# A float32 attention and two MLPs on one core: the early tensors and the second MLP's weights move from the bottom to the top of SBUF

## The reference, cut to what matters

```
q, k, v: (2, 6080, 256) float32; tau: scalar
w_in: (256, 2048), w_out: (2048, 256), once for each of two MLPs

qn = q / (norm(q, axis=1) + 1e-6);  kn = k / (norm(k, axis=1) + 1e-6)
a  = softmax(kn.transpose(0, 2, 1) @ qn / tau)     # 256 x 256 for each batch
x  = (v @ a).reshape(12160, 256)
x  = relu(x @ w_in1)**2 @ w_out1
return relu(x @ w_in2)**2 @ w_out2
```

## Time and profile before

| | |
|---|---|
| median of 3 runs | 2197.22 us (2196.81 to 2197.89) |
| the profiled execution's own time | 2196.81 us |
| its span, first to last instruction | 2194.7 us |
| mean granted TensorE clock | 0.998 |
| TensorE busy | 2179.6 us, 99% |
| VectorE, ScalarE busy | 1252.9 us (57%), 1018.1 us (46%) |

### The profile page before, as it was taken

The page is one execution under the profiler, slowest core; times in us unless marked ns, Lnnn a source line. Parts: engine busy times, 40 slices in busy tenths (PEclk is TensorE's granted clock), DMA queues, the critical chain, the costliest instruction groups (busy, mean ns, idle before and its releaser), DMA issues.

```text
span 2194.7 us, 29614 instructions
## 1 busy us (share of the span) xinstructions
PE 2179.6 (99%) x9836; PEld 1826.6 (83%) x9836; DVE 1252.9 (57%) x1875; ACT 1018.1 (46%) x1722; POOL 3.2 (0%) x10
## 2 busy tenths in 40 slices
PE   8999999999999999999999999999999999999998
PEld 7888888888888888888888888888888888888887
DVE  6765555555565555656655555555555555555544
ACT  5554444444444454444544444444444444444443
POOL 0000000000000000000000000000000000000000
PEclk9999999999999999999999999999999999999999
DMA  8310001100011000112111010110110101101001
GB/s 294 96 49 20 19 19 25 33 19 19 19 29 29 19 19 20 33 23 49 37 20 19 1 20 0 19 19 0 19 18 1 19 0 19 19 0 18 10 1 19
DMA packets 215874, 60.94 MB, mean 28 GB/s; under 512 B 199281, under 2 KB 203377, under 8 KB 215825
## 3 DMA queue, kind: packets, MB, share of 16 engines
q1 hardware_dynamic: 215824, 60.31, 11.7%
HBM read 47.84 MB, written 12.45 MB: 27 GB/s over the span
## 4 chain that ended last, share of the span: by engine, by line
PE 99%; DVE 0%; DMA 0%; ACT 0%; issue 0%; DVEq 0%; SPq 0%
PE bank L321 32%; PE bank L323 32%; PE bank L322 32%; PE bank L455 2%; PE bank L402 0%; DMA qk<-in_k 0%; PE bank L416 0%; DVE s_acc L818 0%; PE bank L410 0%; DVE stats L822 0%; DVE rawl L713 0%; DVE out_sb L726 0%; ACT s_acc L592 0%; ACT rawh L521 0%; DVEq L90 0%
## 5 line engine op out<-in xcount | busy, mean ns | idle before, releaser
L747 DVE TENSOR_TENSOR g_sb<-r_sb 128x512 f32<-128x512 f32 (+1 forms) x768 | 527.3, 687 | 896.6 <-ACT r_sb L545 890.4
L545 ACT ACTIVATE r_sb<-bank 128x512 f32<-128x512 f32 (+1 forms) x768 | 456.0, 594 | 1109.3 <-PE bank L323 1102.1
L713 DVE TENSOR_TENSOR gl<-g_sb,gh 128x512 fp32r<-128x512 f32 (+1 forms) x768 | 519.7, 680 | 0.5 <-DVE g_sb L747 0.5
L533 ACT ACTIVATE gh<-r_sb 128x512 fp32r<-128x512 f32 (+1 forms) x768 | 470.7, 619 | 0.0
L321 PE MATMUL bank<-yh,w2h 128*128 128x512 f32 (+1 forms) x768 | 297.8, 388 | 0.0
L321 PE MATMUL bank<-xh,w1h 128*128 128x512 f32 (+1 forms) x768 | 297.4, 387 | 0.0
L322 PE MATMUL bank<-yl,w2h 128*128 128x512 f32 (+1 forms) x768 | 297.4, 387 | 0.0
L322 PE MATMUL bank<-xl,w1h 128*128 128x512 f32 (+1 forms) x768 | 297.4, 387 | 0.0
L321 PE MATMUL bank<-gh,o2h 128*128 128x512 f32 (+1 forms) x768 | 297.3, 387 | 0.0
L323 PE MATMUL bank<-yh,w2l 128*128 128x512 f32 (+1 forms) x768 | 297.3, 387 | 0.0
L323 PE MATMUL bank<-gh,o2l 128*128 128x512 f32 (+1 forms) x768 | 297.3, 387 | 0.0
(11 more groups left out here) (101 smaller groups left out, 1623.8 us busy)
## 6 DMA issues: line engine op xcount, KB each, us to landing
v_sb<-in_v SPq DMA_DIRECT2D x88, 128.0 KB, 3.0
out<-out_sb SPq DMA_DIRECT2D x88, 128.0 KB, 2.5
raw<-in_q SPq DMA_DIRECT2D x22, 256.0 KB, 2.7
raw<-in_k SPq DMA_DIRECT2D x22, 256.0 KB, 3.0
qk<-in_q SPq DMA_DIRECT2D x10, 512.0 KB, 5.2
qk<-in_k SPq DMA_DIRECT2D x10, 512.0 KB, 6.3
w_early<-in_moe_w_in SPq DMA_DIRECT2D x4, 512.0 KB, 6.0
xT<-in_moe_w_out SPq DMA_DIRECT2D x4, 512.0 KB, 3.9
```

The source lines that it names most:

```text
L533: nc.scalar.activation(gh[:, f % SLOTS, 0:n], r_sb[:, f % 2, 0:n], ACT.Square).then_inc(gh_done, 1)
L545: nc.scalar.activation(r_sb[:, f % 2, 0:n], h_ps[f % SLOTS][:, 0:n], ACT.Relu)\
L713: return nc.vector.tensor_tensor(dst, x, as32(hi), ALU.subtract)
L747: nc.vector.tensor_tensor(g_sb[:, f % 2, 0:n], r, r, ALU.mult).then_inc(sq_done, 1)
```

## The change

One block of allocations is moved behind another. The instructions are the same, row for row, on each engine: 3354 on TensorE, 704 on VectorE, 654 on ScalarE, 14 on GpSimd and 118 on SyncE as the program holds them (loops once), and so are their waits. Only the byte addresses in them differ.

```diff
-        QS, SQ = 4, 2
-        with ExitStack() as early:
-            qk = [sb(f"qk{n}", [P, 2, J * C], scope=early) for n in range(QS)]
-            qk_squares = [sb(f"qk_squares{n}", [P, 2, J * C], scope=early) for n in range(SQ)]
-            w_early = sb("w_early", [P, PIECES, PIECE], scope=early)
-        w2h, w2l = sb("w2h", [P, CB, F], f32r), sb("w2l", [P, CB, F], f32r)
-        o2h, o2l = sb("o2h", [P, NF, C], f32r), sb("o2l", [P, NF, C], f32r)
         w1h, w1l = sb("w1h", [P, CB, F], f32r), sb("w1l", [P, CB, F], f32r)
         o1h, o1l = sb("o1h", [P, NF, C], f32r), sb("o1l", [P, NF, C], f32r)
         xh, xl = sb("xh", [P, CB, TILE], f32r), sb("xl", [P, CB, TILE], f32r)
...
         tau_sb, rtau = stats[:, 0:1], stats[:, 1:2]
         neg_max, row_sum = stats[:, 2:4], stats[:, 4:6]
 
+        QS, SQ = 4, 2
+        with ExitStack() as early:
+            qk = [sb(f"qk{n}", [P, 2, J * C], scope=early) for n in range(QS)]
+            qk_squares = [sb(f"qk_squares{n}", [P, 2, J * C], scope=early) for n in range(SQ)]
+            w_early = sb("w_early", [P, PIECES, PIECE], scope=early)
+        w2h, w2l = sb("w2h", [P, CB, F], f32r), sb("w2l", [P, CB, F], f32r)
+        o2h, o2l = sb("o2h", [P, NF, C], f32r), sb("o2l", [P, NF, C], f32r)
         weights = {"A": (w1h, w1l, o1h, o1l), "B": (w2h, w2l, o2h, o2l)}
```

## The result

The changed kernel takes 2223.77 us, the median of 4 runs (2222.77 to 2223.85), against 2197.01 for the kernel before in 4 runs. The ratio is 1.0121, 95% interval 1.0107 to 1.0136: slower by 26.8 us, where no change was forecast.

What follows compares the result with a forecast made beforehand. TensorE, by the distances between matmul starts, was taken to bound the kernel. Three address terms summed 0 + 0 + 0 against the profiled 2196.81 us, giving a forecast median of 2197.2 us, range 2195.8 to 2198.8.

Steps and rivals of the forecast that it cites:

- The reading of the bound: Whole run: TensorE busy 2179.6 of 2194.7 us, so time is the sum of distances between matmul starts plus 15.1 us.
- The first term: Stages A and B: w1h to o1l and xh to stats move down 65,536 bytes with the same remainders; cost 0.
- The third: Start of the run: first loads of q and k to multiples of 256; taken as 0, bounds -0.3 to +0.6 us.
- The change, part by part: Step pricing three groups of moved addresses, with no instruction added, removed or moved; sum 0 + 0 + 0.
- A faster load gains nothing. Cost: 0: Stages B: w2h to o2l move to the top, on multiples of 256; weight loads are not on the path, 0.
- 106 ns said to be spare: MLP stages: a load takes at most 120 ns and has 226.6 ns to hide in.
- place does not matter: MLP matmuls: w1l and w2l groups share a 389 ns median, so time shows no dependence on where weights are.
- rival (a): Stages B faster: the weights' 128-byte offset may cost 13.3 ns per matmul; 56 us and about 5 more, 2136 us; chance 0.03.
- the forecast of 0.94: Whole kernel: chance given to no measurable change, within about 0.2%, 4.4 us.
- a load is hidden: MLP stages: weight loads hide behind running matmuls with 106 ns to spare, and hidden loads do not stretch a matmul.
- Rival (c): Stages B slower: weight loads of 240 ns would set the matmul distance; 57 us, 2254 us; chance 0.01.
- Rival (b): From 14 to 44 us: slower loads of q and k set the pace; at 25% longer 2203.6 us; chance 0.02.

Runs made afterwards that it cites:

- e9: Kernel before with pads so that only w2l and o2l, low weights of the second MLP, lie 128 bytes off the moving operands; 2215.22 us, ratio 1.0083.
- e2: Kernel before with 128 unused bytes ahead of everything, so every tensor starts on a multiple of 256; 2197.65 us, ratio 0.9998.
- e1: Changed kernel with 128 unused bytes ahead of the early tensors, so w2h to o2l stay at the top, 128 past a multiple of 256; 2196.75 us, ratio 0.9999.
- e11: Kernel before, but the middle matmul of each MLP three uses 64 weight columns, half of that product left out; 2222.75 us in one execution.
- e3: Kernel before with 128 unused bytes ahead of the early tensors and of w1h, so only w2h to o2l start on a multiple of 256; 2223.78 us, ratio 1.0123.
- e5: Kernel before with 128 unused bytes between the weights and xh, so the MLPs' moving operands start on a multiple of 256; 2247.06 us, ratio 1.0225.
- e10: Kernel before with 128 unused bytes ahead of and behind xl, yl and gl, so only these lie 128 off the weights; 2224.57 us, ratio 1.0119.
- e8: Kernel before with pads ahead of w1h and xh, weights 192 bytes past the moving operands in A, 224 in B, modulo 256; 2238.71 us, ratio 1.0194.
- e13: Kernel before with pads ahead of w1h and xh, weights 64 bytes past the moving operands in A, 192 in B, modulo 256; 2234.31 us, ratio 1.0167.

## Why the prediction was wrong

The reading of the bound held: the run is the sum of distances between matmul starts, and 5.7 ns on half of them are the result. The first term (w1h to o1l and the moving operands go down by 65,536 bytes, 0 us) held: A stages kept their pace but for 1.8 us at the borders to B. The third (first loads, -0.3 to +0.6 us) can't be read off the one profile of the changed kernel. The first matmul starts at 4.66 and the DMA share is 0.95 again, but the matmuls of q and k (L455) take 41.3 us and not 40.4, ScalarE's wait for the last tile is 2.36 us and not 2.05, the norms wait 0.24 us for VectorE, and the fold begins 0.8 us later, which is over the upper bound. Most of it lies between 8.6 and 10.7 us, where TensorE started 12 matmuls before and 6 now. That this is the lower clock is likely and not shown: the records of the granted clock begin at 8.5 us before and at 10.8 us now. It is not tied to the addresses: in `e9`, whose early tensors lie where they lay before, it is 6 matmuls too, the q and k matmuls take 41.2 us and the fold begins at 56.87; in `e2`, whose early tensors start on a multiple of 256, they take 40.2 us and it begins at 56.04. With the remainder restored at the same top place (`e1`) the median is 0.6 us under its own before. By all this the term is 0 within the spread of the runs, as forecast.

The rule of the Trainium skill, DMA: Bandwidth & Descriptors, section "How a descriptor splits into AXI transactions", that the prediction named showed no gain for the writes here: 2784 pieces of 4,096 bytes take 159 ns in the median, before and after.

The step that failed is the second, "The change, part by part": "A faster load gains nothing. Cost: 0", with 106 ns said to be spare. It measured +24.6 us (24.1 and 0.5), in the distances of the B matmuls. Two inferences in it were wrong.

The equal rows for w1 and w2 were read as "place does not matter". They are equal because both sets have the same remainder modulo 256, and so had every tensor. The prediction says this in rival (a) and still drew on the rows as the nearest ones. A comparison over places that all share the one property under change has nothing to say on it; the forecast of 0.94 rested on it.

And "a load is hidden" was read as "it costs nothing". The loads' rows changed by at most 1 ns (188 or 189) and the 120 ns of the earlier trace rows stand, but a load that is no longer than before and ends 41 ns ahead of its matmul still goes with a longer distance, after the matmul beside which it runs and after the one that uses it (`e9`). Rival (c) was the right sign and stage at a price of 57 us, through a load of over 226.6 ns that takes over the pace. Its mechanism is not what the rows show: the loads stayed at 188 ns, and in `e11` the run was slower with a load of 134 ns. Rival (a), that the 13.3 ns over 512 / 2.4 come from the remainder of 128, is refuted by `e2`, where every start is a multiple of 256 and the pace is the same. Rival (b) did not occur.

The Trainium skill, TensorE: Matmul & The Clock Gate, section "Step-by-step: what each phase is for", says that TensorE reads SBUF through two independent ports and that loading the next weights does not steal bandwidth from the running matmul. The result is hard to fit with that in this kernel: relative addresses alone change the pace (226.8 ns at distance 0, 232.5 at 128; `e1`, `e2`, `e3`, `e5`), so load and stream do meet somewhere. That they meet in the reads of SBUF is not shown.

What stays open is how load and stream meet, and whether the stream is slowed or the next start is held back; distances between starts can't tell. Each distance in bytes settles into a short pattern that repeats: 227, 226, 227 ns at 0 (226.7 in the mean, 544 cycles of 2.4 GHz), 231 and 236 in turn at 64, 237, 231, 232 at 160. At 192, and in `e10`, there are two such patterns at the same addresses. A phase between loads and streams that locks in at one of a few values would fit all of this; it is argued, not shown. Whether distances that are no multiple of 32 bytes matter was not tried. Nothing that was run beats the kernel before.

## What to carry to other kernels

Where float32r matmuls of 512 columns follow each other without a gap and each has its own weight load, keep the start of the weights and the start of the moving operands equal modulo 256 bytes, and check this whenever an allocation is added or moved: here moving one block behind a 128-byte tensor cost 1.2%, and distances of 32 and 64 bytes 2.6%. For other widths measure it first: with 448 columns the best distance here was another one. Look for it in the distances between starts in a window with no idle time. Before the trace is taken as proof that something doesn't matter, ask whether that thing varies in it at all.

## What the hardware showed that was not expected

For 512 columns only the relative start counts: 226.8 ns at distance 0 with both on a multiple of 256 or both 128 past one, 229.5 to 230.3 at 192 (a mix of 228.9 and 233.3), and 232.4 to 234.3 at 32, 64, 96, 128, 160 and 224. In the stages with 448 columns the same 128 bytes cost 1.4 ns and not 5.7 (204.0 against 202.6), 224 bytes cost 3.9 (206.5), and 192 bytes gain 2.3 to 2.5 ns (200.3 in A of `e8`, 200.2 in B of `e13`): there 0 is not the best distance. A middle matmul of 64 weight columns in place of 128 slowed the whole by 25 us, though its load's row fell from 0.19 to 0.13 us.
